# Turning the next pair's q, k and tails one step earlier, and moving one normalise ahead of the masks

## What is computed

```python
# attention: 4 batches x 8 heads, 576 rows, head size 64
scores = scale * np.matmul(q, k.transpose(0, 1, 3, 2))
thresh = np.max(scores, axis=-1, keepdims=True) - tau
scores = np.where(scores >= thresh, scores, -1000000000.0)
scores = scores - np.max(scores, axis=-1, keepdims=True)
attn = np.exp(scores)
attn = attn / (np.sum(attn, axis=-1, keepdims=True) + 1e-09)
attn_out = np.matmul(attn, v)
...
# experts: 2304 tokens of 512, logits against 8 embeddings, argmax, h = relu(x @ w1[e]), gate * (h @ w2[e])
# dense: h = x @ w_in; g = max(h, 0) + alpha * min(h, 0); out = g @ w_out
```

## Time and profile before

| | |
|---|---|
| median of 3 runs | 1011.72 us (1011.56 to 1011.73) |
| profiled execution, its own time | 1013.92 us |
| span of the profiled execution | 1012.2 us |
| mean granted TensorE clock | 0.997 |
| TensorE busy | 1001.4 us, 99% of the span |
| weight loads busy | 886.6 us, 88% |
| VectorE busy | 529.3 us, 52% |
| ScalarE busy | 388.9 us, 38% |
| GpSimd busy | 337.6 us, 33% |

### The profile page before, as it was taken

The page is one execution under the profiler, slowest core; times in us unless marked ns, Lnnn a source line. Parts: engine busy times, 40 slices in busy tenths (PEclk is TensorE's granted clock), DMA queues, the critical chain, the costliest instruction groups (busy, mean ns, idle before and its releaser), DMA issues.

```text
span 1012.2 us, 19467 instructions
## 1 busy us (share of the span) xinstructions
PE 1001.4 (99%) x6541; PEld 886.6 (88%) x6542; DVE 529.3 (52%) x1206; ACT 388.9 (38%) x814; POOL 337.6 (33%) x446
## 2 busy tenths in 40 slices
PE   9999999999999999999999999999999999999997
PEld 8999999999998788888888889999899999998996
DVE  5888888888988422222222237544444434444442
ACT  5777777777776232222232223211121211111111
POOL 2233344222131789999854542010010100100101
PEclk9999999999999999999999999999999999999999
DMA  5876777776671655566563435001001000000000
GB/s 124 222 166 168 189 192 176 189 191 164 157 190 42 219 196 195 206 213 205 181 198 129 130 126 160 1 32 32 1 32 32 32 15 17 31 0 0 32 1 31
DMA packets 103744, 116.69 MB, mean 115 GB/s; under 512 B 70380, under 2 KB 70412, under 8 KB 103156
## 3 DMA queue, kind: packets, MB, share of 16 engines
q1 hardware_dynamic: 88404, 87.52, 31.6%
q10 hardware_dynamic: 11120, 13.97, 4.4%
q0 software_dynamic: 4144, 14.20, 4.0%
HBM read 68.53 MB, written 19.12 MB: 87 GB/s over the span
## 4 chain that ended last, share of the span: by engine, by line
PE 95%; POOL 2%; DVE 1%; issue 1%; DMA 0%; ACT 0%; POOLq 0%; SPq 0%; DVEq 0%
PE bank L790 82%; PE bank L793 13%; POOL ring L690 1%; DVE neg_max L1563 0%; POOL ring L688 0%; DMA qraw<-in_q 0%; DVE probs L1571 0%; POOLq L89 0%; POOL out L783 0%; POOL x_sorted L731 0%; DVE X L1602 0%; ACT probs L1302 0%; ACT o_row L1527 0%; DVE emb_row L1757 0%; DVE X L1652 0%
## 5 line engine op out<-in xcount | busy, mean ns | idle before, releaser
L790 PE MATMUL bank<-x_hi,ring 128*128 128x384 f32 x768 | 210.7, 337 | 0.0
L790 PE MATMUL bank<-ring,g_hi 128*128 128x512 f32 x576 | 179.2, 392 | 0.0
L1504 ACT ACTIVATE g_hi<-act 128x384 fp32r<-128x384 f32 x96 | 50.4, 525 | 299.2 <-DVE act L1947 296.7
L690 POOL TENSOR_TENSOR ring<-stage,ring 128x2048 fp32r<-128x2048 f32 x32 | 147.2, 4600 | 4.8 <-POOL ring L688 0.2
L790 PEld LDWEIGHTS bank<-x_hi,ring 128*128 128x128 f32 x768 | 140.3, 188 | 3.5
L1944 DVE TENSOR_SCALAR neg<-bank,alpha_col 128x384 f32<-128x384 f32 x96 | 59.2, 617 | 150.9 <-PE bank L790 150.9
L790 PE MATMUL bank<-x_lo,ring 128*128 128x384 f32 x384 | 129.0, 336 | 0.0
L1302 ACT ACTIVATE probs<-bank,neg_max 128x576 f32<-128x576 f32 x144 | 102.8, 741 | 59.4 <-DVE neg_max L1563 59.4
L790 PEld LDWEIGHTS bank<-ring,g_hi 128*128 128x128 f32 x576 | 106.9, 188 | 18.6 <-DVE g_lo L1895 0.3
L1571 DVE SCALAR_TENSOR_TENSOR probs<-bank,thresh,probs 128x576 f32<-128x576 f32 x144 | 112.7, 816 | 14.2 <-ACT probs L1302 13.6
L1563 DVE TENSOR_REDUCE neg_max<-bank 128x1 f32<-128x576 f32 x144 | 104.1, 754 | 25.1 <-PE bank L790 24.2
(11 more groups left out here) (204 smaller groups left out, 1412.7 us busy)
## 6 DMA issues: line engine op xcount, KB each, us to landing
stage<-in_moe_w SPq DMA_DIRECT2D x26, 1024.0 KB, 5.3
k_st<-k_both SPq DMA_DIRECT2D x60, 288.0 KB, 5.2
x_row<-x_sorted ACTq DMA_DIRECT2D x23, 296.0 KB, 3.3
stage<-in_moe_w SPq DMA_DIRECT2D x12, 512.0 KB, 6.2
y_sorted<-y_row ACTq DMA_DIRECT2D x21, 256.5 KB, 2.9
q_st<-q_hi SPq DMA_DIRECT2D x30, 160.0 KB, 2.8
q_st<-q_lo SPq DMA_DIRECT2D x30, 160.0 KB, 2.9
qraw<-in_q SPq DMA_DIRECT2D x16, 256.0 KB, 3.3
```

The source lines that it names most:

```text
L690: nc.gpsimd.tensor_tensor(lo, src, hi.bitcast(F32), ALU.subtract).then_inc(piece_lo, 2)
L790: return nc.tensor.matmul(dst, lhsT, rhs, start=start, stop=stop)
L1504: nc.scalar.activation(g_hi[f % 3][:, :], act2[f % 2][:, :], ACT.Copy).then_inc(g_hi_ready, 1)
```

## The change

Two edits. `group_of` gives, from pair 1 on, the groups to steps 1, 2 and 3 and not to steps 2, 3 and 4. Pair 0 keeps its steps, so pair 2's tails are still turned in step 4 of pair 0 and split in step 0 of pair 1. And in step 0 of pairs 1 to 14 `normalise` stands ahead of the masks, as it does in all other steps.

```diff
             if (n, j) == (0, 0):
                 return 1, 2
-            m, g = n + 2, j - 2
-            return (m, g) if g >= 0 and m < PAIRS else None
+            m, g = n + 2, j - (1 if n else 2)
+            return (m, g) if 0 <= g < GROUPS_PREP and m < PAIRS else None
...
-                    late = j == 0 and 0 < n < PAIRS - 1
-                    if not (static(n) and j < 4) and not late:
+                    if not (static(n) and j < 4):
                         normalise(*((n, j - 4) if j >= 4 else (n - 1, j + UNITS - 4)))
...
                     for h in heads_of(n, j):
                         mask(n, j, h)
-                    if late:
-                        normalise(n - 1, UNITS - 4)
```

## The result

| | before | after |
|---|---|---|
| median of five runs | 1011.72 us (1011.56 to 1011.73) | 1016.11 us (1015.54 to 1017.28) |
| profiled execution, its own time | 1013.92 us | 1015.54 us |
| span of the profiled execution | 1012.2 us | 1013.8 us |

The change makes the kernel slower: a ratio of 1.0045, with a 95% interval of 1.0032 to 1.0059. That is 4.4 us by the medians, where 0.3 was forecast and 1014.6 was the upper end of the range.

A forecast was written before the change was run, and what follows sets the result against it. TensorE was taken to bound the kernel, with VectorE holding it up in places. Terms -1.0 + 0.25 + 0.3 - 0.3 + 1.0 = +0.25 us took the median from 1011.72 to 1012.0, range 1009.0 to 1014.6.

The forecast's parts named there:

- Pair 1: +1.0 us: In pair 1, ScalarE's k split waits 1.8 us for pair 2's spread; TensorE loses 1.0, between 0 and 1.8.
- the rest is q's split waiting for its own spread: Pair 1, ScalarE: part of the 0.6 us shift of the exponentials of step 3, put down to q's split waiting.
- nothing hides any of it: Upper end of the pair 1 loss: TensorE feels the whole 1.8 us wait for the spread of k.
- Pair 14: This pair has no turn to pay and keeps the whole 0.29 us gain: -0.3 us.
- The steady pair: A plain pair takes 19.35 us against 19.43, so 0.08 gained; over pairs 2 to 13, -1.0 us.
- Pair 12: A routing step of 0.76 comes on top of q's split on VectorE: +0.25 us, between 0 and 0.5.
- Pairs 6 and 10: TensorE's small ranking products in step 0 lose the time they hid in: +0.15 us each, 0.3 in sum.
- Pairs 2 to 13 together: Twelve pairs at -1.0 us, with +0.25 for the routing step and +0.3 for the ranking products.
- The split of the gain: Per pair, 0.29 us gained as normalise and tail splits leave step 0's end, less 0.22 for the tails' uncovered turn.
- The 2.7 us: Comparison estimate for 288 KB of one spread of k, by about 2 us plus bytes at 436 GB/s; it gives 1011.0.
- Rival 3: Slower: ScalarE's k split waits for its spread in every pair, 0.4 us each in twelve pairs; 1016.5 us, chance 0.14.
- Rival 2: No wait in pair 1, since the spread lands before 48.1; 1011.0 us, chance 0.12.

The follow-up runs named there:

- late-opening profile: The changed kernel run again unchanged, profiled in an execution with scores of (1,0) at 33.56: 1018.28 us where before had 1013.94, ratio 1.0045.
- the groups alone: Against the changed kernel, the normalise of step 0 goes back behind the masks while the groups stay in steps 1 to 3: 1015.36 us, ratio 1.0041.
- the kernel with the step of 9.88: The changed kernel with the copy to x_row issued by SP, not ScalarE, run on one chip beside the changed kernel: 1017.87 us, ratio 1.0036.
- the last experiment: The changed kernel with groups moved only from pair 2 on, SP's two transfers in pass 1, and x_row copied by SP: 1015.43 us, ratio 1.0013.
- the two runs without a wait of q: The changed kernel with a weight chunk and blank rows issued behind pair 2's spreads (1013.96 us), or without pair 3's raw q and k loads (1013.82 us).
- the run without raw loads: The changed kernel without SP's loads of raw q and k of pair 3, computed from pair 1's rows instead: 1013.82 us, ratio 0.9997.

## Why the prediction was wrong

**The step that failed** is "Pair 1: +1.0 us", and in it the sentence that took q's split, "the rest is q's split waiting for its own spread", as some 0.5 on ScalarE and nothing on TensorE. The mechanism named for k was the right one, an ask one step earlier for a buffer that is still being spread, but the wait was q's, 3.28 and not 0.5, and it cost 4.2. Four things made the difference:

- *The phase of the profiled execution, 1.0.* TensorE opened 2.3 late in it, and SP's spreads of pair 2 started only 1.3 late (39.35 against 38.04). So it showed 1.0 more room between the spread and the ask than most profiled executions have. Its own time, 2.2 above the median, stood in the table, and was used for the sum only. The late-opening profile of the changed kernel, with 0.26 for q and 1.99 for k, shows that the reading was sound for that phase, as far as one profile can.
- *The landing, 1.7.* The prediction gives no landing for q; its 0.5 amounts to some 2.9 after the last issue (an estimate from the earlier trace rows and the exponentials of step 2 at 42.23 to 43.72). From that issue to ScalarE's split it was 4.6 in the changed kernel (39.89 to 44.49), 4.5 in the groups alone and in the kernel with the step of 9.88, 3.1 in the late opening (40.77 to 43.83) and 3.0 in pair 2 of the last experiment (60.42 to 63.42). For k both ends, 3.4 and 6.0, were carried through; for q no range was kept. In the two runs without a wait of q it was at most 3.05 and 3.6, so the earlier issue was not all that these edits brought.
- *The cover.* TensorE was put behind ScalarE's k by way of VectorE's low part and the tails' turn. In the traces it stops earlier, at `turn_out`, which needs ScalarE's copies behind the split. Only some 0.5 to 0.7 of a wait is hidden, counted by the length of the step: 3.32 becomes 2.78, 2.08 becomes 1.41, 1.04 becomes 0.36.
- *The clock, 0 to 2.7.* After idle times of 2.49, 2.00 and 2.80 TensorE worked at half clock (steps of 8.35, 7.80 and 9.88; in the second the clock fell 1.4 after it had started again), after 2.52, 2.27 and 2.10 at full clock throughout (6.89, 6.63 and 6.45). The 2.7 is an estimate: 9.88 less 4.11, less the 3.05 that a wait of 3.59 costs with 0.54 hidden. Such a term was not in the sum at all; its upper bound of 1.8, "nothing hides any of it", fell for this reason too.

**Pair 14**, forecast at -0.3, came at +0.3. Step 4 of pair 13 and steps 0 and 1 gave 0.4 back, and step 2 lost 0.6 to ScalarE's wait for the scatter. With SP issuing the copy this loss is gone (3.70, 3.68 and 3.67 in three runs), on the third chip from 5.38 to 3.68 side by side, so the wait is shown. Its size is not fixed: 3.77 to 5.38 for this step in the six profiles with moved groups and the copy on ScalarE. Why the scatter lands later is only argued: SP, no longer held, issues the spreads of pair 15 at its side, 4.4 earlier than before.

**What held.** The steady pair: block of steps 4 and 0 6.96 to 6.97 for a forecast 7.04, steps 4.12 to 4.13, 4.11 to 4.13 and 4.08 to 4.09 for 4.12, 4.12, 4.07. Pair 12: 19.61 against 19.44, +0.17, where +0.25 less 0.08 stood. Pairs 6 and 10 were +0.19 each, not +0.07. Pairs 2 to 13 together: -0.6 for -0.45. The split of the gain was wrong, though: 0.29 was credited to the normalise and the tails' splits together, and 0.22 charged for the tails' turn. Alone, the normalise gives 0.20 a pair, and the groups alone give 0.14, all that both give together.

**One price.** The 2.7 us that the prediction works out for comparison is for one transfer of 288 KB. k's spread is four of them, 1152 KB, in flight together, so the 3.4 to 6.0 of the earlier trace rows neither confirms nor refutes it.

**The rivals.** Rival 3 named the mechanism of a spread that binds, and the side, but "in every pair". In the changed kernel it binds once, in the first pair with the new order; after that SP is one step ahead and the wait is gone, as the forecast said. Where the order moves from pair 2 on, k still waits in the next one or two pairs (0.99; 0.91 and 0.54). That the rival's 1016.5 is near the measured 1016.11 is luck: the reason was another. Rival 2, no wait in pair 1, is what the run without raw loads imitates.

## What to carry to other kernels

An operation that is moved one step earlier asks for its buffer one step earlier in the first round too, before the queue that serves it has had a round to get ahead; work out that first round alone, with the longest landing in the trace, and for every operation that moves. Where the profiled execution's own time is off the median by as much as the effect looked for, its slack between two engines is one sample; take the room as smaller by up to the whole of that difference (here 1.0 of 2.2). Here the small edit was the good one: the normalise ahead of the masks gives 0.998, with two early transfers of SP put behind the spreads 0.9967 and 0.9978, and the moved groups take that away.

## What the runs showed of the hardware

- Idle times of TensorE of 2.0 to 2.8 us are followed by a granted clock of 0.50 in three executions and stay at 1.00 in three others (2.49 and 2.52 fell on different sides), and the low clock lasted from some 3 us to over 6. A wait of that size has no single price.
- The same spread of q, four transfers of 160 KB each in one queue, took 3.0 to 4.6 us from the last issue to the waiting engine.
- In the second and third batches the kernel before took 1014.23 and 1013.94 us and in the first 1011.73. Between the profile read for the prediction and that of the second batch half of it stands in pairs 2 and 3, and half around pair 14: step 4 of pair 13 and step 0 of pair 14, 3.50 and 3.61 in the first, are 4.22 and 4.12 in the second. Whether it is the chip is left open.
